# Preparing the first pair of chunks: norms from the token layout, 32x32 diagonal products of their own, beta applied after the inverse, and four banks for the second pair's gram products

## The chip, the cores and the metric

The kernel runs on one core of a Trainium2 chip. A core has a matrix engine (TensorE, PE in the profile), a vector engine (VectorE, DVE), a scalar engine (ScalarE, ACT), a general engine (GpSimd, POOL), and a fifth one that mostly issues transfers (SyncE, SP). Each runs its own list of instructions in order and waits on semaphores that the others raise. PE writes into eight PSUM banks of 128 x 512 floats; the other tiles lie in SBUF. The metric is the device time of one execution in microseconds (us), lower is better.

## The reference

Three stages: a delta-rule attention over 768 steps for 4 batches of 8 heads with head size 48, then two feed-forward stages over 3072 tokens.

```python
k_n = k / (np.linalg.norm(k, axis=-1, keepdims=True) + 1e-06)
for t in range(S):
    kt, vt, bt = (k_n[:, :, t], v[:, :, t], beta[:, :, t, None])
    y[:, :, t] = np.einsum('bhd,bhde->bhe', q[:, :, t], state)
    v_old = np.einsum('bhde,bhd->bhe', state, kt)
    state = state + bt[:, :, :, None] * np.einsum('bhd,bhe->bhde', kt, vt - v_old)
...
x = y.transpose(0, 2, 1, 3).reshape(B * S, H * D)
x = (x @ w_a) * (x @ w_b) @ w_out          # 384 -> 1536 -> 384
h = x @ w_in                               # 384 -> 2048
return (np.maximum(h, 0) + alpha * np.minimum(h, 0)) @ w_out2
```

## The kernel before

The sequence of 768 steps is cut into 12 chunks of T = 64 steps, handled in six pairs. Within a chunk the recurrence becomes a triangular system per head: the Gram products of the chunk's keys, scaled by beta, give a 64 x 64 matrix. The inverses of its 32 x 32 diagonal blocks are computed by VectorE alone, for all heads of both chunks at once: `IN` (a 32 x 32 block transpose `blk<-dgc`), 34 steps `ROW`, and `XT` (the transpose `xt<-inv`). After that the chain of small products `H2`, `H3`, `H4`, `HS`, `HY`, `H1` carries the state from chunk to chunk.

The rows of a pair's tokens for four batches form one tile of 512 tokens. The feed-forward stages of tile i run on PE as long three-part products (a high and a low half of each float), while the attention of pair i+1 is fitted in beside them. The first pair has no tile to lie beside: everything until the first unit `A` of tile 0 stands in front of it. This report is about that opening part.

One list, `seq`, holds the steps of the whole kernel in one order, and each engine walks through it and issues what is its own of every step. So the order of each engine's instructions is written by hand. The steps of the opening that the text speaks of:

- `LTK`, `LTQ` p b load keys and queries of pair p, batch b, with tokens on partitions and both heads of a pair side by side (`k_tok`, `q_tok`); `LK` loads keys in a second layout (`k_raw`), in which a chunk's tokens stand where the chain wants them. `WL` loads feed-forward weights.
- `SQ`, `KS`, `KN`, `KI` make the norms: square on ACT, sum on DVE, square root on ACT, and on DVE the reciprocal and its product with beta (`beta_all`).
- `BP`, `B` bring all beta values and alpha to partitions with 96 tiny products and one transpose on PE, and copy them out on ACT.
- `TRK`, `TRQ` transpose keys and queries of the first pair through the banks `att`, and ACT copies them to `kq0` and `kz0`. `TR` does the same for pair 1.
- `GK` c hf is the Gram product of the keys of chunk c, half hf of the heads; DVE multiplies it by beta into `gs`. `DG0` copies the 32 x 32 diagonal blocks out of `gs` to `dgc`, half on DVE, half on ACT. `GQ` is the product of keys and queries, `PT` its masking on DVE. `GG` c g makes both kinds for the chunks 2 and 3 of pair 1, in the two banks `att`; ACT copies them out.
- `VS` scales v by the norm on POOL. `GM` multiplies a `gs` by beta in place.
- `F` is a product of constants (`warm`), whose result nobody reads. It keeps PE busy.

PE and ACT work through `TR` and `GG` while DVE inverts; the chain's first product, `H2` of chunk 0, comes behind all of them in PE's list. A 32-bit product of the opening counts as two matmuls in the profile, a transpose and an `F` as one.

## Time and profile before

| | us |
|---|---|
| median of 3 runs | 1048.64 (1048.0 to 1048.91) |
| the profiled execution, its own time | 1048.36 |
| its span in the trace | 1046.6 |
| PE busy | 1020.3 (97% of the span) |
| DVE busy | 570.5 (55%) |
| ACT busy | 407.4 (39%) |
| first matmul of tile 0 | starts at 84.66 |

All times in the text are microseconds from the start of the span unless they are durations. An instruction's row gives its start, its time, its engine and line, what it writes and reads, how many instructions the row merges, and in brackets how long the engine sat idle before it and what ended that. PEclk is the granted share of the full clock of PE: 1.00 is 2.4 GHz and 0.50 is 1.2 GHz. After 84.66 PE is busy nearly without a break until the end.

### The profile page before, as it was taken

The page shows a single profiled execution, that of the slowest core. Times are in us where ns is not written, and L with a number is a line of the kernel's source. Part 1 is how long each engine was busy: PE and PEld are TensorE (multiplying, and loading weights), DVE is VectorE, ACT ScalarE, POOL GpSimd, SP SyncE. Part 2 cuts the span into 40 slices and gives each one's busy share as a digit, 9 for nine tenths or more (in the row PEclk, how much of TensorE's full clock was granted, in tenths as well). Part 3 has the DMA queues.
Part 4 walks back from the last instruction along what each step waited for, and adds up shares of the span by engine and source line. Part 5 has one row for each costly group of instructions (what it writes and reads, how often), then busy time and mean ns, then how long its engine had stood idle before and what let it go on. Part 6 is the DMA issues. An engine that isn't in the chain of part 4 may idle for free.

```text
span 1046.6 us, 24293 instructions
## 1 busy us (share of the span) xinstructions
PE 1020.3 (97%) x10240; PEld 853.1 (82%) x10240; DVE 570.5 (55%) x888; ACT 407.4 (39%) x774; POOL 113.5 (11%) x111
## 2 busy tenths in 40 slices
PE   6789999999999999999999999999999999999998
PEld 4557888898887888787889788889888888888898
DVE  5975876544687343496445477544368643322333
ACT  4425335564313344422434332435432334312433
POOL 4013663441000000000001000001000000000000
PEclk9899999999999999999999999999999999999999
DMA  9627998778875556696457596556556446766562
GB/s 159 127 64 224 305 325 265 240 247 277 223 228 168 164 166 218 182 251 185 147 159 233 157 249 208 154 167 205 173 177 194 144 150 185 224 194 195 182 191 81
DMA packets 191739, 203.82 MB, mean 195 GB/s; under 512 B 109392, under 2 KB 139168, under 8 KB 191632
## 3 DMA queue, kind: packets, MB, share of 16 engines
q1 hardware_dynamic: 188000, 200.73, 64.7%
q8 instruction: 82, 1.34, 0.6%
q0 software_dynamic: 576, 0.93, 0.5%
q10 hardware_dynamic: 3056, 0.61, 0.3%
q14 instruction: 25, 0.20, 0.1%
HBM read 166.04 MB, written 31.46 MB: 189 GB/s over the span
## 4 chain that ended last, share of the span: by engine, by line
PE 93%; ACT 3%; DVE 1%; issue 1%; DMA 1%; ACTq 0%; SPq 0%; DVEq 0%
PE bank L470 28%; PE bank L472 27%; PE bank L471 27%; PE bank L555 2%; PE bank L499 1%; PE bank L653 1%; PE bank L574 1%; PE bank L602 1%; PE bank L605 1%; PE bank L618 1%; PE bank L599 1%; ACT kz L770 1%; PE bank L647 1%; PE bank L650 1%; PE bank L563 1%
## 5 line engine op out<-in xcount | busy, mean ns | idle before, releaser
L877 ACT CAST g_hi<-g_sb 128x512 fp32r<-128x512 f32 x168 | 104.2, 620 | 249.2 <-DVE g_sb L1139 158.0
L470 PE MATMUL bank<-x_hi,w_two 128*128 128x512 f32 x432 | 171.2, 396 | 1.1 <-DVE x_lo L1128 1.1
L1144 DVE SCALAR_TENSOR_TENSOR g_sb<-f_sb,neg_alpha,e_sb 128x512 f32<-128x512 f32 x96 | 73.5, 766 | 177.7 <-ACT f_sb L874 177.0
L472 PE MATMUL bank<-x_hi,w_two 128*128 128x512 f32 x432 | 168.5, 390 | 0.0
L471 PE MATMUL bank<-x_lo,w_two 128*128 128x512 f32 x432 | 168.5, 390 | 0.0
L1150 DVE TENSOR_TENSOR g_lo<-g_sb,g_hi 128x512 fp32r<-128x512 f32 x168 | 121.0, 720 | 79.4 <-ACT g_hi L877 79.1
L472 PE MATMUL bank<-w_two,g_lo 128*128 128x384 f32 x384 | 129.2, 337 | 0.0
L470 PE MATMUL bank<-w_two,g_hi 128*128 128x384 f32 x384 | 129.1, 336 | 0.0
L471 PE MATMUL bank<-w_two,g_hi 128*128 128x384 f32 x384 | 128.8, 335 | 0.0
L1139 DVE TENSOR_TENSOR g_sb<-e_sb,bank 128x512 f32<-128x512 f32 x72 | 49.4, 686 | 140.8 <-PE bank L472 140.5
L470 PE MATMUL bank<-m_hi,w_two 128*128 128x512 f32 x288 | 118.1, 410 | 0.1
L471 PE MATMUL bank<-m_lo,w_two 128*128 128x512 f32 x288 | 113.6, 394 | 0.0
L472 PE MATMUL bank<-m_hi,w_two 128*128 128x512 f32 x288 | 113.2, 393 | 0.0
L873 ACT ACTIVATE e_sb<-bank 128x512 f32<-128x512 f32 x96 | 57.4, 598 | 132.5 <-PE bank L472 132.4
L866 ACT COPY e_sb<-bank 128x512 f32<-128x512 f32 x72 | 42.4, 588 | 149.0 <-PE bank L472 148.9
L470 PEld LDWEIGHTS bank<-x_hi,w_two 128*128 128x128 f32 x432 | 81.1, 188 | 19.1 <-issue 2.9
L472 PEld LDWEIGHTS bank<-x_hi,w_two 128*128 128x128 f32 x432 | 81.1, 188 | 17.2
L471 PEld LDWEIGHTS bank<-x_lo,w_two 128*128 128x128 f32 x432 | 81.2, 188 | 15.9
L1212 POOL TENSOR_TENSOR w_two<-w_ring,w_two 128x384 fp32r<-128x384 f32 x68 | 79.6, 1187 | 92.5 <-ACT w_two L853 92.4
L470 PE MATMUL bank<-g_hi,w_two 128*128 128x512 f32 x216 | 85.8, 397 | 0.3 <-DVE g_lo L1150 0.3
L471 PE MATMUL bank<-g_lo,w_two 128*128 128x512 f32 x216 | 84.3, 390 | 0.0
L472 PE MATMUL bank<-g_hi,w_two 128*128 128x512 f32 x216 | 84.2, 390 | 0.0
(143 smaller groups left out, 1536.5 us busy)
## 6 DMA issues: line engine op xcount, KB each, us to landing
w_two<-split_scratch SPq DMA_DIRECT2D x340, 384.0 KB, 3.5
split_scratch<-w_two SPq DMA_DIRECT2D x68, 384.0 KB, 4.3
w_ring<-in_moe_w_out_dram SPq DMA_DIRECT2D x28, 192.0 KB, 4.0
k_tok<-in_k_dram SPq DMA_DIRECT2D x24, 192.0 KB, 4.8
q_tok<-in_q_dram SPq DMA_DIRECT2D x24, 192.0 KB, 4.7
out_dram<-o_sb SPq DMA_DIRECT2D x24, 192.0 KB, 3.5
w_ring<-in_moe_w_in_dram SPq DMA_DIRECT2D x16, 192.0 KB, 3.9
x_raw<-y_sb SPq DMA_DIRECT2D x30, 96.0 KB, 2.4
```

Source lines behind the costliest of these rows:

```text
L470: pe.matmul(dst, lhs_hi, rhs_hi, start=start, stop=False)
L471: pe.matmul(dst, lhs_hi, rhs_lo, start=False, stop=False)
L472: return pe.matmul(dst, lhs_lo, rhs_hi, start=False, stop=stop)
L499: mm = pe.transpose(bk[:, j, i], src[:, 2 * g + j].rearrange("p h t -> p (h t)"), ident[:])
L555: mm = pe.matmul(bk[hf][tok(hf, h), 2 * T * j:2 * T * (j + 1)].rearrange("p (i t) -> p i t", t=T), kt(p, hf, w, e, rows), both, start=True ...
L866: act.copy(e_sb[:, f % 2], h_bank[0][:, :]).then_inc(e_ok, 1)
L873: act.activation(e_sb[:, f % 2], h_bank[f % 2][:, :], ACT.Relu).then_inc(e_ok, 1)
L877: act.copy(g_hi[:, j % GR], g_sb[:, j % GR]).then_inc(gh_ok, 1)
L1139: dve.tensor_tensor(g_sb[:, j % GR], e_sb[:, f % 2], h_bank[1][:, :], ALU.mult).then_inc(g_ok, 1)
L1144: dve.scalar_tensor_tensor(g_sb[:, j % GR], f_sb[:, f % 2], neg_alpha[:, f:f + 1], e_sb[:, f % 2], ALU.mult, ALU.add).then_inc(g_ok, 1)
L1150: dve.tensor_tensor(g_lo[:, s], g_sb[:, s], g_hi[:, s].bitcast(F32), ALU.subtract).then_inc(gl_ok, 1)
L1212: pool.tensor_tensor(w_lo[:, r], w_raw[:, r], w_hi[:, r].bitcast(F32), ALU.subtract).then_inc(lo_ok, 1)
```

## The change

- Norms of the first pair come from `k_tok`, by new steps `KS0` on DVE (square and sum, batch by batch as it lands), and `KP` on PE, which brings the sums to the chunk layout with 12 small products; `KN` takes the root from PSUM. `k_raw` of pair 0 is loaded later, behind the second pair's `LTQ`, and all of it by SP. The loads of `k_tok` and `q_tok` of pair 0 are shared by SP and ACT; POOL issues beta's.
- `GD` makes the 32 x 32 diagonal blocks by 128 products of their own (64 for each half), and `DG0` is now one DVE multiply by beta for each half, from PSUM to `dgc`. ACT copies the `GK` results to `gs` without beta, and `GM` 0 and 1 put beta in behind the inverse.
- `BP0` brings beta of the first two chunks only. The other 80 products of `BP`, alpha's transpose and the copies `B` move behind `GQ`.
- `GG` for chunk 3 uses two further banks (`spare`), and the six `F` between `GG` steps go. Sixteen `F` stand before `H2` of chunk 0, in four groups that wait for a step of the inverse each and for ACT's last copy from `spare`.
- `PT` of the first pair moves behind `H3` of chunk 0 and `H2` of chunk 1 in DVE's list, and `GM` 1 stands before DVE's part of `H1` of chunk 1.
- Two memsets of banks on DVE go, and one of `su` moves from DVE to POOL.

The diff, cut to its core:

```diff
+        spare, kn_bank, b0_bank = (bank[0], bank[2]), bank[3], bank[5]
...
-        seq = [("LK", 0, 0)] + [("LTK", 0, b) for b in range(B)] + [("LTQ", 0, b) for b in range(B)]
-        seq += [("BP",)] + [("F", 0)] * 8 + flat(norms(0)[:2]) + [("B",)] + flat(norms(0)[2:])
-        seq += [("TRK", 0)] + [("F", 0)] * 3 + [("TRK", 1)] + [("F", 0)] * 3 + [("GK", 0, 0), ("GK", 1, 0)]
-        seq += [("TRK", 2), ("TRK", 3)] + [("F", 0)] * 3 + [("DG0", 0), ("GK", 0, 1), ("GK", 1, 1), ("DG0", 1), ("IN", 0)]
+        seq = [("LTK", 0, b) for b in range(B)] + [("LTQ", 0, b) for b in range(B)]
+        seq += [("F", 3)] * 8 + [("KS0", 0), ("TRK", 0), ("F", 3), ("F", 3), ("KS0", 1), ("TRK", 1), ("BP0",), ("GD", 0)]
+        seq += [("KS0", 2), ("KS0", 3), ("TRK", 2), ("TRK", 3), ("KP",), ("KN", 0), ("GK", 0, 0), ("GD", 1), ("GK", 1, 0)]
+        seq += [("GK", 0, 1), ("GK", 1, 1), ("KI", 0), ("DG0", 0), ("DG0", 1), ("IN", 0)]
         seq += [("LTK", 1, b) for b in range(B)] + [("LTQ", 1, b) for b in range(B)]
-        seq += [("LK", 1, 0), ("LK", 1, 1)] + [("WL", n) for n in range(RG)] + [("VS", 0), ("VS", 1)]
-        seq += [("TRQ", b) for b in range(B)] + [("GQ", 0), ("GQ", 1), ("GC",)]
+        seq += [("LK", p, j) for p in range(2) for j in range(2)] + [("WL", n) for n in range(RG)] + [("VS", 0), ("VS", 1)]
+        seq += [("TRQ", b) for b in range(B)] + [("GQ", 0), ("GQ", 1), ("GC",), ("BP",), ("B",)]
         for g in TR_ORDER:
-            seq += [("TR", 1, g)] + [("F", 0)] * (2 * (g >= 4))
+            seq += [("TR", 1, g)] + [("F", 3)] * (2 * (g >= 4))
         for g in range(2):
             for c in (2, 3):
-                seq += [("GG", c, g)] + [("F", 0)] * (2 if (c, g) == (3, 1) else 6)
+                seq += [("GG", c, g)]
         seq += [("SQ", 2)]
         for n in range(1, ROWS + 1):
             seq += [("ROW", 0, n)]
-        seq += [("XT", 0)] + [("F", R16 + 14)] * 4 + [("F", ROWS)] * 8
-        seq += [("PT", 0, 0), ("PT", 0, 1)]
-        beside0 = {(0, "H2"): [("KS", 2), ("SQ", 3)], (0, "H4"): [("KS", 3), ("KN", 1)], (0, "HS"): [("KI", 1), ("LV", 2)],
-                   (0, "HY"): [("XL", 0, 0, T)], (1, "H1"): [("PT", 1, 0), ("PT", 1, 1), ("WS", 0)], (1, "H2"): [("WS", 1)],
-                   (1, "H3"): [("WS", 2)], (1, "H4"): [("GM", 2), ("GM", 3), ("WS", 3), ("WT", 0), ("WT", 1)]}
+        seq += [("XT", 0)] + [("F", 0, R16 + 8)] * 4 + [("F", 0, R16 + 12)] * 4 + [("F", 0, R16 + 14)] * 4 + [("F", 0, ROWS)] * 4
...
+        seq += [("GM", 0)]
+        beside0 = {(0, "H2"): [("KS", 2), ("SQ", 3)], (0, "H3"): [("PT", 0, 0), ("PT", 0, 1)], (0, "H4"): [("KS", 3), ("KN", 1)],
+                   (0, "HS"): [("KI", 1), ("LV", 2)], (0, "HY"): [("XL", 0, 0, T), ("GM", 1)], (1, "H1"): [("WS", 0)],
+                   (1, "H2"): [("PT", 1, 0), ("PT", 1, 1), ("WS", 1)], (1, "H3"): [("WS", 2)],
+                   (1, "H4"): [("GM", 2), ("GM", 3), ("WS", 3), ("WT", 0), ("WT", 1)]}
...
+                    if p == 0 and b % 2:
+                        continue
                     if p == 1:
                         sp.wait_ge(*is_full(b % 2, "TRK" if kind == "LTK" else "TRQ", b))
+                        if kind == "LTK":
+                            sp.wait_ge(ks0_ok, b + 1)
...
+                elif kind == "GD":
+                    hf = st[1]
+                    for b in range(2):
+                        pe.wait_ge(*is_free(b, "TRK", 2 * hf + b))
+                    for j in range(UH):
+                        for c in range(2):
+                            n = SB * (UH * c + j)
+                            for i in range(2):
+                                for h, rows in enumerate(LOW):
+                                    x = kt(0, hf, j, c, rows)[:, SB * i:SB * i + SB]
+                                    mm = pe.matmul(spare[hf][quad(2 * (h ^ hf) + i), n:n + SB], x, x, start=True, stop=True)
+                    mm.then_inc(gd_full, 1)
+                elif kind == "BP0":
+                    pe.wait_ge(beta_ld, 32)
+                    for c in range(2):
+                        mm = beta_quarters(b0_bank, c)
+                    mm.then_inc(b0_full, 1)
+                elif kind == "KP":
+                    pe.wait_ge(ks0_ok, B)
+                    for c in range(2):
+                        for h in range(2):
+                            pe.matmul(kn_bank[tok(0, h), c * U:c * U + UH], ident[:, c * T:c * T + T], ksum_tok[:, units(0), h],
+                                      start=True, stop=True)
+                            for i in range(2):
+                                mm = pe.matmul(kn_bank[quad(2 * (1 - h) + 1 - i), c * U + UH:c * U + U],
+                                               ident[:, c * T + SB * i:c * T + SB * i + SB], ksum_tok[:, units(1), h],
+                                               start=True, stop=True)
+                    mm.then_inc(kp_full, 1)
...
+                    if (c, hf) == (1, 0):
+                        pe.wait_ge(b0_ok, 1)
+                    elif (c, hf) == (1, 1):
+                        pe.wait_ge(kn_ok, 1)
...
+                    pe.wait_ge(dgv_ok, 2)
...
+                    if c == 3:
+                        if g:
+                            pe.wait_ge(sp_free, 2)
+                        bk, filled = spare, (sp_full, sp_full)
+                    else:
+                        bk, filled = in_banks(*st), full
...
-                    pe.wait_ge(vinit, 3)
                     if st[1]:
-                        pe.wait_ge(solve, st[1] + 1)
-                    pe.matmul(bank[0][:, :], warm[:, 0:P], warm[:], start=True, stop=True)
+                        pe.wait_ge(vinit, 2)
+                    else:
+                        pe.wait_ge(sp_free, 4)
+                        pe.wait_ge(solve, st[2] + 1)
+                    pe.matmul(bank[st[1]][:, :], warm[:, 0:P], warm[:], start=True, stop=True)
...
+                    if kind == "H3" and c < 2:
+                        pe.wait_ge(gm0_ok, c + 1)
...
-            for h in range(2):
-                act.dma_start(beta_rows[:, :, HALVES[h]], beta.rearrange("b (u two) (c t) -> two (b u) c t", two=2, t=T)[h]
-                              ).then_inc(beta_ld, 16)
-            load_k(act, 0, 1)
+            for kind in ("LTK", "LTQ"):
+                for b in range(1, B, 2):
+                    load_tok(act, kind, 0, b)
...
+                elif kind == "GK":
+                    _, c, hf = st
+                    act.wait_ge(gk_full, 2 * hf + c + 1)
+                    act.copy(gs(c)[:, units(hf), :].rearrange("p w t -> p (w t)"), g0_bank[2 * c + hf][:, :]).then_inc(gk_free, 1)
...
-                elif kind == "DG0":
-                    hf = st[1]
-                    act.wait_ge(gk_free, 2 * hf + 2)
-                    for i in range(2):
-                        for c in range(2):
-                            ins = act.copy(dgc[quad(i), c * U + UH * hf:c * U + UH * hf + UH, :],
-                                           gs(c)[quad(i), units(hf), SB * i:SB * i + SB])
-                    ins.then_inc(dg_ok, 1)
...
-            for x in y0_bank:
-                dve.memset(x[:, :], 0.0)
...
+                if kind == "KS0":
+                    b = st[1]
+                    dve.wait_ge(kt_ld[b], 16)
+                    x = k_tok[:, UQ * b:UQ * b + UQ, :, 0:D]
+                    dve.tensor_tensor(squares0(b), x, x, ALU.mult).then_inc(sq0_ok, 1)
+                    dve.wait_ge(sq0_ok, b + 1)
+                    dve.tensor_reduce(ksum_tok[:, UQ * b:UQ * b + UQ], squares0(b), AX.X, ALU.add).then_inc(ks0_ok, 1)
+                elif kind == "TRK" and st[1] == 3:
+                    dve.wait_ge(*is_full(1, *st))
+                    src = att[1][:, :].rearrange("p (w e t) -> p w e t", e=2, t=T)
+                    for i in range(2):
+                        ins = dve.tensor_copy(kz0[:, UQ:UH, :, 0, SB * i:SB * i + SB], src[:, :, :, SB * (1 - i):SB * (1 - i) + SB])
+                    ins.then_inc(free[1], 1)
...
+                    if c < 2:
+                        dve.wait_ge(gk_free, 4)
+                        dve.tensor_tensor(gs(c)[:], gs(c)[:], beta_all[:, c].unsqueeze(2).to_broadcast([P, U, T]), ALU.mult
+                                          ).then_inc(gm0_ok, 1)
+                        continue
...
-                elif kind == "GK":
-                    _, c, hf = st
-                    dve.wait_ge(gk_full, 2 * hf + c + 1)
+                elif kind == "DG0":
+                    hf = st[1]
+                    dve.wait_ge(gd_full, hf + 1)
                     dve.wait_ge(ki_ok, 3)
-                    dve.tensor_tensor(gs(c)[:, units(hf), :], g0_bank[2 * c + hf][:, :].rearrange("p (w t) -> p w t", t=T),
-                                      beta_all[:, c, units(hf)].unsqueeze(2).to_broadcast([P, UH, T]), ALU.mult
-                                      ).then_inc(gk_free, 1)
-                elif kind == "DG0":
-                    hf = st[1]
-                    dve.wait_ge(gk_free, 2 * hf + 2)
-                    for i in (2, 3):
-                        for c in range(2):
-                            ins = dve.tensor_copy(dgc[quad(i), c * U + UH * hf:c * U + UH * hf + UH, :],
-                                                  gs(c)[quad(i), units(hf), SB * (i - 2):SB * (i - 2) + SB])
-                    ins.then_inc(dgv_ok, 1)
+                    dve.tensor_tensor(dgc[:].rearrange("p (c u) t -> p c u t", c=2)[:, :, units(hf)],
+                                      spare[hf][:, :].rearrange("p (c u t) -> p c u t", c=2, t=SB),
+                                      beta_all[:, 0:2, units(hf)].unsqueeze(3).to_broadcast([P, 2, UH, SB]), ALU.mult
+                                      ).then_inc(dgv_ok, 1)
...
-            pool.dma_start(alpha_rows[:], alpha.rearrange("(f p) -> f p", p=P)).then_inc(al_ld, 16)
+            for h in range(2):
+                pool.dma_start(beta_rows[:, :, HALVES[h]], beta.rearrange("b (u two) (c t) -> two (b u) c t", two=2, t=T)[h]
...
-            pool.wait_ge(gk_full, 2)
+            pool.wait_ge(gq_full, 1)
```

The program's list of PE from its start up to the transposes of the queries, before (L538 and L541 are `BP`, L563 `F`, L508 `TRK` and `TRQ`, L516 `GK`):

```order
L538 MATMUL bank<-ident,y_sb 32x8 x96
L541 MATMUL bank<-ident,alpha_rows 128x16
L563 MATMUL bank<-warm 128x512 x8
L508 MATMUL bank<-ident,k_tok 128x128 x4
L563 MATMUL bank<-warm 128x512 x3
L508 MATMUL bank<-ident,k_tok 128x128 x4
L563 MATMUL bank<-warm 128x512 x3
L516 MATMUL bank<-kq 64x64 x32
L508 MATMUL bank<-ident,k_tok 128x128 x8
L563 MATMUL bank<-warm 128x512 x3
L516 MATMUL bank<-kz 64x64 x32
L508 MATMUL bank<-ident,q_tok 128x128 x16
```

The same stretch of PE's list in the changed program (L494 is `BP0`, L546 `GD`, L558 and L561 `KP`, L575 `GK`, L533 the transposes, L629 `F`):

```order
L533 MATMUL bank<-ident,k_tok 128x128 x4
L494 MATMUL bank<-ident,y_sb 32x8 x16
L546 MATMUL bank<-kq 32x32 x64
L533 MATMUL bank<-ident,k_tok 128x128 x8
L558 MATMUL bank<-ksum_tok,ident 64x8
L561 MATMUL bank<-ksum_tok,ident 32x8 x2
...
L575 MATMUL bank<-kq 64x64 x16
L546 MATMUL bank<-kz 32x32 x64
L575 MATMUL bank<-kq 64x64 x16
L575 MATMUL bank<-kz 64x64 x32
L533 MATMUL bank<-ident,q_tok 128x128 x16
```

The 96 products of `BP` have left the head of the list but for 16; `GD` and `KP` add 140 between the first transposes and the queries' ones.

DVE's list from the last transpose of the inverse on, before (L977 is `XT`, L1067 and L1073 `PT`, L1085 `H2`, L988 `KS`, L1099 `H3`, L1105 `H4`):

```order
L977 STREAM_TRANSPOSE xt<-inv 128x32x32
L1067 TENSOR_TENSOR pt_0<-bank,upper 128x512
L1073 TENSOR_TENSOR kz<-bank,upper 64x8x64 x2
L1085 COPY w_sb<-bank 128x384
L988 TENSOR_REDUCE ksum<-k_sq 128x16
L1099 TENSOR_TENSOR r_sb<-r_sb,bank 128x384 x2
L1105 TENSOR_TENSOR u_sb<-bank,beta_all 128x384
```

And in the changed program (L1049 is `XT`, L1099 `GM`, L1175 `H2`, L1073 `KS`, L1189 `H3`, L1157 and L1163 `PT`, L1195 `H4`):

```order
L1049 STREAM_TRANSPOSE xt<-inv 128x32x32
L1099 TENSOR_TENSOR gs_0<-gs_0,beta_all 128x1024
L1175 COPY w_sb<-bank 128x384
L1073 TENSOR_REDUCE ksum<-k_sq 128x16
L1189 TENSOR_TENSOR r_sb<-r_sb,bank 128x384 x2
L1157 TENSOR_TENSOR pt_0<-bank,upper 128x512
L1163 TENSOR_TENSOR kz<-bank,upper 64x8x64 x2
L1195 TENSOR_TENSOR u_sb<-bank,beta_all 128x384
```

`PT` has moved from before the chain into it, between `H3` and `H4`, and `GM` 0 stands where `PT` was.

PE's list behind `GQ` in the changed program (L494 and L598 are `BP`, L523 `TR`); before, the `TR` rows followed `GQ` directly:

```order
L588 MATMUL bank<-kz 64x64 x2
L494 MATMUL bank<-ident,y_sb 32x8 x80
L598 MATMUL bank<-ident,alpha_rows 128x16
L523 MATMUL bank<-ident,k_tok 128x2x64
L523 MATMUL bank<-ident,q_tok 128x2x64
```

The 80 products now stand between the last product of the first pair and everything that pair 1 needs.

## Rows read from the trace of the kernel before

**Rows 1.** The page: span, and the queue of instruction blocks (blocks, MB, share).
```profile
span 1046.6 us, 24293 instructions
...
q8 instruction: 82, 1.34, 0.6%
```

**Rows 2.** DVE in order of time: start, time, what, idle before and its releaser.
```profile
22.41 1.97 DVE L920 STREAM_TRANSPOSE blk<-dgc 128x1024 f32<-128x1024 f32 x1 [0.28 <-ACT dgc L791]
...
49.61 2.09 DVE L977 STREAM_TRANSPOSE xt<-inv 128x1024 f32<-128x1024 f32 x1
51.62 0.64 DVE L1067 TENSOR_TENSOR pt<-bank,upper 128x512 f32<-128x512 f32 x1
52.28 1.39 DVE L1073 TENSOR_TENSOR kz<-bank,upper 64x512 f32<-64x512 f32 x2
...
59.63 0.56 DVE L1105 TENSOR_TENSOR u_sb<-bank,beta_all 128x384 f32<-128x384 f32 x1 [1.22 <-PE bank L605]
...
71.10 1.02 DVE L1099 TENSOR_TENSOR r_sb<-r_sb,bank 128x384 f32<-128x384 f32 x2 [1.43 <-PE bank L602]
...
74.81 2.34 DVE L1013 TENSOR_TENSOR gs<-gs,beta_all 128x1024 f32<-128x1024 f32 x2
```

**Rows 3.** PE in order of time, the opening.
```profile
4.54 2.74 PE L538 MATMUL bank<-ident,y_sb 16*32 16x8 f32 x192 [4.54 <-DMA y_sb<-in_beta_dram]
...
7.43 3.59 PE L563 MATMUL bank<-warm 128*128 128x512 bf16 x8
...
14.06 2.15 PE L516 MATMUL bank<-kq 48*64 48x64 f32 x64
...
32.22 0.37 PE L528 MATMUL bank<-kz 48*64 48x64 f32 x2 [2.83 <-issue]
...
33.27 0.47 PE L499 MATMUL bank<-ident,k_tok 128*128 128x128 f32 x1
...
51.68 3.19 PE L563 MATMUL bank<-warm 128*128 128x512 bf16 x14
54.81 0.88 PE L599 MATMUL bank<-r_sb,xt 32*32 32x48 f32 x64
...
70.76 0.36 PE L602 MATMUL bank<-w_sb,gs 32*32 32x48 f32 x12 [0.15 <-issue]
...
76.16 0.26 PE L650 MATMUL bank<-pt,u_sb 64*48 64x64 f32 x2 [0.24 <-issue]
```

**Rows 4.** ACT in order of time.
```profile
9.29 0.84 ACT L742 ACTIVATE k_sq<-k_raw 128x768 f32<-128x768 f32 x1 [2.31 <-DMA k_raw<-in_k_dram]
...
23.74 2.37 ACT L784 COPY kz<-bank 64x512 f32<-64x512 f32 x4 [0.32 <-PE bank L508]
...
40.90 0.74 ACT L770 COPY kz<-bank 64x256 f32<-64x256 f32 x2
...
51.77 0.37 ACT L808 COPY gs<-bank 128x256 f32<-128x256 f32 x1 [1.27 <-PE bank L555]
...
52.71 0.75 ACT L813 COPY kz<-bank 64x256 f32<-64x256 f32 x2
```

**Rows 5.** Stretches: busy us (count) of PE, PEld, DVE, ACT, POOL; PEclk, DMA, GB/s.
```profile
0.00:29.40 29.40, 20.19 (x471) 15.30 (x471) 18.26 (x41) 11.95 (x25) 11.27 (x28) 0.93 1.12 159
...
0.00:70.70 70.70, 53.14 (x1216) 36.44 (x1217) 53.40 (x88) 31.09 (x73) 16.65 (x33) 0.93 0.69 115
0.00:76.15 76.15, 56.77 (x1342) 38.62 (x1343) 57.35 (x95) 31.09 (x73) 18.09 (x34) 0.93 0.67 118
```

**Rows 6.** DMA queues in 8.4:8.6, 16.4:16.6, 28.8:29, 59.8:60: blocks, MB, share.
```profile
q8 instruction: 1, 0.02, 44.3%
...
q8 instruction: 1, 0.02, 45.5%
...
q8 instruction: 1, 0.02, 53.3%
...
q8 instruction: 1, 0.02, 28.8%
```

120 lines of the change are left out of this document (77 added, 43 removed).

## The prediction

> **What bounds the kernel now.** I read the page first, then the engines' rows in order of time from 0 to 90, then the stretches, then the DMA queues. PE is busy without a break from 84.66 on, and the change leaves every instruction after that point as it is. So only the start of tile 0 can move, and the end moves with it, one to one. The opening ends in a chain of small products whose first, `H2` of chunk 0, starts at 54.81 [rows 3]. Everything between that and 84.66 hangs on it.
>
> Two strands meet at `H2`. The first is DVE: the inversion starts at 22.41 with the transpose to `blk` and ends with `xt` at 51.70, 29.3 us in which DVE waits for nobody [rows 2]. The second is PE and ACT in turn: `TR` from 33.27 [rows 3], ACT's last `TR` copy at 41.64, and four rounds of `GG`, of which ACT has the last copied out at 53.46 [rows 4]. PE then works off 14 `F` from 51.68 to 54.8 [rows 3]. `H2` starts as the last `F` ends, 3.1 us after `xt` is there. So the second strand is the later one: from the start of `TR` to `H2` it takes 54.81 - 33.27 = 21.5 us. The reader should also see the halt of 2.83 us at 32.22, within `GQ`, which the trace lays to "issue" [rows 3]: PE waited for no engine there, and it delays `TR` in full.
>
> **That halt is the key of this forecast.** Three PE rows of the opening have an idle time laid to "issue": 32.22, 70.76 and 76.16 [rows 3]. The matmuls recorded before them are 471, 1216 and 1342 [rows 5]. The distances are 745 and 126; 745 is 6 times 124. The page has 82 instruction blocks fetched [rows 1], and 10240 matmuls over 82 is 125. So PE's program comes in blocks of about 125 matmuls (each with its weight load), and the halts fall on the borders between blocks. Blocks are fetched by the same DMA engines as the data. Borders lie near matmul 98 (within `BP`, 4.54 + 98 x 2.74/192 = 5.9), 223 (14.3), 350 (19.9) and 471 (29.4). Block transfers start at about 8.5, 16.5, 28.9 [rows 6]: 2.5, 2.1 and 9.0 us behind the first three borders. The share of the stretch times 0.2 times 16 gives their lengths: 1.4, 1.5, 1.7. The halt ended at 32.22, 1.6 after the third transfer. This fits a fetch that is asked for at one border and needed at the next. From asking to having it took 2.5 + 1.4 + 1.6 = 5.5, then 5.2, then 12.3 us. Later, with the DMA engines nearly idle, the border at 58.7 has its transfer at 59.9, 0.9 long [rows 6]: 1.2 + 0.9 + 1.6 = 3.7 us. A block must therefore last 4 to 5 us, or PE stands still. The kernel before has one such halt, because its 193 matmuls of `BP` come first and `F` and waits stretch the rest.
>
> The Trainium skill ("Runtime: NRT & Kernel Launch", Instruction fetch mechanics) says blocks have 256 instructions, are fetched while the previous one runs, and that crossing a border is "mostly hidden"; it gives PE room for eight blocks. The block size agrees with this trace (125 matmuls and as many loads); the hiding does not, at 32.22, with its 2.83 us. By the skill's rule the halts would all be absent; the first rival below is that case.
>
> **The change part by part.** Start of the inversion. `F` runs from about 2.7 (the memsets of two banks, 1.0 us, are gone from DVE), 3.6 us for eight [rows 3]; the first transposes and two `F` end at 9.0. The keys have 192-byte pieces as before, where ACT had all of `k_raw` at 9.29 behind beta [rows 4]; now they are first in two queues, so about 5 to 8: no wait. `GD` 0 starts at 9.8. One `GK` pair of 64 matmuls takes 2.15 [rows 3]; `GD` has 128 matmuls, of a kind the trace does not show. `BP` gives 14.3 ns each, `H2` (32x32) 13.8, `GK` 34; `GD` uses four parts of the array at once like `H2`, so I take 14.3: 1.8 us for each half, 1.7 to 4.3 as bounds. Norms take DVE 4 x 1.1 us beside this and end at about 10. Without halts `GD` 1 ends at 15.9 and the inversion starts at 16.7, 5.7 us sooner than 22.41.
>
> With borders at the same spacing, they fall in the changed program at matmul 96 (the 46th of `GD` 0), 223 (13 matmuls into `GK`), 348 (the 106th of `GD` 1), 474 (the end of the second `TRQ`), 598 (near the end of `GQ`) and 724 (the 114th of the 160 of `BP`).
> - First border 9.8 + 46 x 0.0143 = 10.4. The DMA engines carry keys and queries as they did at 8.5. Block ready 5.5 later, 15.9, against 13.5 without a halt.
> - Second border 15.9; by then the loads have run dry (SP waits for `TRQ`), so 3.7: 19.6, against 18.1. `GD` 1 ends at 19.9 and the inversion starts at 21.0, `xt` is ready at 50.3.
> - From 19.6: rest of `GD` 1 0.3, three `GK` 3.2, `TRQ` with ACT's copies (two of 0.59, then 2.37 for four [rows 4]) to 27.7, `GQ` up to the 598th matmul 1.8: fifth border at 29.5. The one between, at 24.1, was asked for at 19.6 and costs nothing.
> - At 29.5 queries of pair 1, `k_raw` and v are in flight. Block ready 5.2 later (the second fetch of before; 3.7 to 12.3 as bounds): 34.7. Without a halt that border comes at 31.7. Then the rest of `BP`, alpha and ACT's `B`: 1.6.
> - `TR` starts at 36.3, against 33.27: +3.0 us. With no halts at all it would start at 28.6, since `BP` itself puts 2.4 us and `B` 0.5 in front of it.
>
> From `TR` to `H2`. Before 21.5. `TR` is ACT's time, 8.3 from 33.27 to 41.64. `GG` before took 11.8, from 41.64 to 53.46; with four banks ACT's copies follow each other, 1.70 each (51.77 to 53.46 [rows 4]), 4 x 1.70 + 1.1 for the first product + 0.1 of gaps = 8.0. The sixteen `F` wait for the last of them (`sp_free` 4): 16 x 3.13/14 = 3.6 us, all behind it, since three of their four steps of the inverse are past. Sum 8.3 + 8.0 + 3.6 = 19.9, so -1.6 us. `H2` is then at 56.2, behind `xt` (50.3) and `GM` 0, which is hidden.
>
> From `H2` to tile 0. `PT` stands between `H3` and `H4` on DVE: it frees at 58.4 (59.63 less the idle 1.22), plus 2.03 for `PT` [rows 2] is 60.5, against 59.63: +0.85. In chunk 1 `GM` 1 (2.34 / 2 = 1.17) and `PT` stand in front of `r_sb`; `PT` has left the place before `w_sb`, and the step at 71.10 comes at 71.7: +0.6. Together +1.45; bounds 0 (if the loads before tile 0 cover it) and 3.2 (2.03 + 1.17, all in series).
>
> Sum: +3.0 - 1.6 + 1.45 = +2.85 us. The profiled execution took 1048.36, of which the span is 1046.6, so 1051.2; it lay 0.3 under the median of the runs, so I say 1051.4.
>
> **Rivals.**
> - A: no halts. For: between 40 and 84 the halts are 0.24 at most [rows 3]. Against: 32.22. `TR` at 28.6 is -4.7, with -1.6 and +1.45 makes -4.85: 1043.8. (This is the case of the rule quoted from the Trainium skill.) If `GD` and the small products run still quicker, 1042.5.
> - B: short halts, 3.7 us for every block. Second border 14.1, third 17.8, `GQ`'s 27.6, `BP` continues at 31.3, `TR` at 32.9: -0.4 - 1.6 + 1.45 = -0.5: 1048.1. No measurable change.
> - C, slower: my forecast. It decides from the point where the three exposed fetches sum to over 12 us (`TR` later than 33.4); here 5.5 + 3.7 + 5.2 = 14.4.
> - D: a fetch behind `GQ` like the third of before, 12.3 us, with PE at half clock in `TR` after the halt: `TR` at 43.4, +10: 1058.
> - E: `k_raw` of pair 1 lands late, 24 loads being issued by SP alone after `LTQ`. I expect them by 48 and ACT's square after 52; it costs nothing unless PE runs without halts, then up to 1 us.
>
> **How the numbers follow.** 0.43 for C with 1049.8 to 1055, 0.03 for D, 0.22 for B (within 0.2%, 2.1 us, which is about what a measurement of this kernel can tell from no change) and 0.32 for A with what lies between it and B. C's own range is 1049.5 to 1055.5. For all, the range is 1043.4 to 1055.3: A's end leaves out about a tenth, D and the far end of C another. Faster 0.32, same 0.22, slower 0.46. The likeliest single case is C, 1051.4.
>
> **What would show it.** In the changed profile: idle times laid to "issue" of 1 to 3 us in `GK` (L575) after 13 matmuls and late in the second `GD` (L546), and one of 3 us or more within the 160 matmuls of L494; the inversion's transpose at 21 (not 16.7); `TR` at 36; ACT's `GG` copies back to back; sixteen `F` in one piece of 3.6 us before `H2`. I am wrong if the halts are missing or under 1 us in sum, if `TR` starts before 31, or if `F` is spread over the inverse's steps, which would say that the second strand was ahead of DVE.

## The result, and the profile after

| | before | after |
|---|---|---|
| median of the runs made together | 1048.32 (4 runs, 1046.83 to 1048.91) | 1061.03 (4 runs, 1060.78 to 1061.81) |
| ratio, 95% interval | | 1.0125 (1.0107 to 1.0142) |
| span of the profiled execution | 1046.6 | 1059.0 |
| first matmul of tile 0 | 84.66 | 97.41 |

The change makes the kernel slower by 1.25%. The forecast was 1051.4, with 1043.4 to 1055.3 as range: the sign came out, and halts for instruction blocks are there as forecast, but the size did not come out, and the result lies outside the range. From tile 0 to the end both need the same time (961.9 and 961.6), so the whole loss is in the opening. Split at the points that the prediction uses:

| us | before | after | difference | forecast |
|---|---|---|---|---|
| start of `TR` | 33.27 | 41.00 | +7.7 | +3.0 |
| from there to the first `GG` | 8.5 | 9.1 | +0.6 | 0 |
| from there to ACT's last `GG` copy | 11.7 | 7.6 | -4.1 | -3.8 |
| from there to `H2` of chunk 0 | 1.4 | 5.8 | +4.4 | +2.2 |
| from there to tile 0 | 29.85 | 33.99 | +4.1 | +1.45 |
| sum | 84.66 | 97.41 | +12.75 | +2.85 |

PE of the changed kernel in order of time (the columns are those of [rows 3], which these rows answer):

```profile
12.86 0.50 PE L575 MATMUL bank<-kq 48*64 48x64 f32 x9
16.66 1.54 PE L575 MATMUL bank<-kq 48*64 48x64 f32 x23 [3.30 <-issue]
18.14 1.64 PE L546 MATMUL bank<-kz 48*32 48x32 f32 x105
20.22 0.54 PE L546 MATMUL bank<-kz 48*32 48x32 f32 x23 [0.44 <-issue]
...
22.41 2.83 PE L575 MATMUL bank<-kz 48*64 48x64 f32 x58
...
29.98 0.27 PE L588 MATMUL bank<-kq 48*64 48x64 f32 x2 [2.27 <-ACT kz L864]
...
34.48 0.37 PE L588 MATMUL bank<-kq 48*64 48x64 f32 x2 [2.14 <-issue]
...
35.12 1.68 PE L494 MATMUL bank<-ident,y_sb 16*32 16x8 f32 x112
39.40 0.83 PE L494 MATMUL bank<-ident,y_sb 16*32 16x8 f32 x48 [2.61 <-issue]
...
41.00 0.45 PE L523 MATMUL bank<-ident,k_tok 128*128 128x128 f32 x1 [0.56 <-ACT neg_alpha L815]
...
57.72 5.77 PE L629 MATMUL bank<-warm 128*128 128x512 bf16 x16 [1.74 <-ACT kz L888]
63.42 0.88 PE L667 MATMUL bank<-r_sb,xt 32*32 32x48 f32 x64
...
72.34 1.95 PE L723 MATMUL bank<-kz,su 128*48 128x64 f32 x32
...
84.01 0.88 PE L673 MATMUL bank<-r_sb,xt 32*32 32x48 f32 x64 [2.59 <-DVE r_sb L1189]
```

The reader sees four halts laid to "issue" in place of the one of before: 3.30 behind the ninth of the first `GK`, 0.44 behind the 105th of the second `GD`, 2.14 in `GQ`, 2.61 behind the 112th of the late `BP`. Together 8.5 us. Three stand where the block borders were forecast (13th, 106th, 114th matmul). The sixteen `F` take 5.77 us, not 3.6.

The granted clock in four stretches (PE, PEld, DVE, ACT, POOL busy with counts; PEclk; DMA share; GB/s), against which before has 1.00 until 22 and from 38 on:

```profile
14.00:18.00 4.00, 1.34 (x23) 1.33 (x22) 0.96 (x3) 0.00 (x0) 0.00 (x0) 0.54 0.86 124
18.00:22.00 4.00, 3.56 (x154) 3.25 (x155) 1.08 (x2) 0.58 (x1) 0.00 (x0) 0.50 0.02 4
...
38.00:42.00 4.00, 2.04 (x54) 1.94 (x55) 3.79 (x7) 0.38 (x2) 1.12 (x2) 0.50 0.85 161
...
58.00:62.00 4.00, 4.00 (x11) 1.36 (x10) 0.00 (x0) 0.41 (x1) 0.00 (x0) 0.50 0.04 9
```

DVE, answering [rows 2]. The inversion starts at 21.61, and its second half of diagonals had waited 5.71 us for PE:

```profile
20.82 0.69 DVE L1147 TENSOR_TENSOR dgc<-bank,beta_all 128x512 f32<-128x512 f32 x1 [5.71 <-PE bank L546]
21.61 1.95 DVE L992 STREAM_TRANSPOSE blk<-dgc 128x1024 f32<-128x1024 f32 x1
...
48.88 2.11 DVE L1049 STREAM_TRANSPOSE xt<-inv 128x1024 f32<-128x1024 f32 x1
...
79.55 0.68 DVE L1157 TENSOR_TENSOR pt<-bank,upper 128x512 f32<-128x512 f32 x1
80.26 2.67 DVE L1163 TENSOR_TENSOR kz<-kz,upper 64x512 f32<-64x512 f32 x2
82.86 1.00 DVE L1189 TENSOR_TENSOR r_sb<-r_sb,bank 128x384 f32<-128x384 f32 x2
```

ACT's copies of `GG` ([rows 4]) now follow one another, and the last ends at 57.66:

```profile
51.20 0.37 ACT L883 COPY gs<-bank 128x256 f32<-128x256 f32 x1 [1.27 <-PE bank L618]
...
56.92 0.74 ACT L888 COPY kz<-bank 64x256 f32<-64x256 f32 x2
```

### The profile page after: what moved, and what is told of

The parts are those of the page before. It is cut to its first block, busy times and chain, and to the rows that moved or that the text cites. A ratio compares the mean times of both kernels' runs of the same rounds, so it can differ in the third digit from the quotient of the medians.

```text
span 1059.0 us, 24861 instructions
## 1 busy us (share of the span) xinstructions
PE 1025.0 (97%) x10497; PEld 859.2 (81%) x10497; DVE 572.9 (54%) x885; ACT 404.4 (38%) x768; POOL 117.8 (11%) x114
## 4 chain that ended last, share of the span: by engine, by line
PE 93%; ACT 2%; issue 2%; DVE 1%; DMA 1%; SPq 0%; POOL 0%; DVEq 0%; ACTq 0%; POOLq 0%
PE bank L486 28%; PE bank L488 26%; PE bank L487 26%; PE bank L618 2%; PE bank L523 1%; PE bank L723 1%; PE bank L640 1%; PE bank L667 1%; PE bank L688 1%; PE bank L673 1%; PE bank L670 1%; PE bank L629 1%; ACT kz L850 1%; PE bank L717 1%; DMA y_sb<-in_beta_dram 1%
```

## The experiments

Every time of a milestone below is from the profiled execution of its kernel. The kernel before was run beside each set: medians of 1048.52, 1047.01, 1047.72 and 1047.57 us. Its 13 runs beside the first set lie between 1046.06 and 1051.61, so a difference of 1 or 2 us between kernels that ran once says little by itself; there the milestones within the trace carry the argument.

**Do halts move with the number of products?** Three kernels add work to the kernel before. In two of them the added product is one of `BP`'s kind, in the third an `F`, and nobody reads what they write. All diffs below are cut to the lines of `seq` and the few others that matter.

b_shift, 32 tiny products in front (64 recorded matmuls, half a block):

```diff
-        seq += [("BP",)] + [("F", 0)] * 8 + flat(norms(0)[:2]) + [("B",)] + flat(norms(0)[2:])
+        seq += [("SM", 4), ("BP",)] + [("F", 0)] * 6 + flat(norms(0)[:2]) + [("B",)] + flat(norms(0)[2:])
```

> The kernel before with 32 more tiny products (64 matmuls) in front of BP and two F fewer; 62 matmuls are added ahead of everything. Theory 1 (a block of about 125 matmuls is asked for at one border and needed at the next): the halt within GQ moves from the 101st recorded matmul of GQ to about the 40th, and the two small halts of H3 and HY in chunk 1 move about 62 matmuls earlier too. Theory 2 (the halts belong to a place or a time, such as the loads of v or a bank in use): the halt stays at the same product of GQ or at the same time, 29.4. The time changes by less than 2 us either way.

Measured 1053.33 (one run), tile 0 at 89.74. The halt in `GQ` is gone, and a new one stands in `BP`, behind its 158th matmul, which is the 222nd of the program, where the second border lies:

```profile
5.46 2.32 PE L538 MATMUL bank<-ident,y_sb 16*32 16x8 f32 x158
11.14 0.65 PE L538 MATMUL bank<-ident,y_sb 16*32 16x8 f32 x34 [3.35 <-issue]
```

The little halts of [rows 3] moved too, about 60 matmuls to the front. So a halt belongs to a place in the instruction stream. Whether there is one, and how long, depends on how soon PE gets there: here 222 tiny matmuls are over within 3.2 us, and before the same border was passed at 14.3 without a halt. Two things were not as the first theory had them: no halt stands at the 40th matmul of `GQ`, and the time grew by some 5 us (tile 0 by 5.1) and not by under 2.

b_small80, 80 tiny products between `GQ` and `TR`, where the change puts the late `BP`:

```diff
-        seq += [("TRQ", b) for b in range(B)] + [("GQ", 0), ("GQ", 1), ("GC",)]
+        seq += [("TRQ", b) for b in range(B)] + [("GQ", 0), ("GQ", 1), ("GC",), ("SM", 10)]
```

> The kernel before with 80 tiny products (160 matmuls, the same kind as BP) between GQ and TR, where the changed kernel has BP. Their own time is 2.3 us. Theory 1: they use up more than a block within 2.3 us, so a further halt of 2 to 5 us appears inside them at about the 97th matmul; TR starts 4.5 to 7 us later than 33.3. Theory 2 (only the time in PE's list counts): TR starts 2.3 us later and no halt appears.

b_long6, six `F` in the same place:

```diff
+        seq += [("TRQ", b) for b in range(B)] + [("GQ", 0), ("GQ", 1), ("GC",)] + [("F", 0)] * 6
```

> The kernel before with six F in the same place as the 80 tiny products of the other run: 6 matmuls instead of 160, at 0.22 to 0.43 us each 1.3 to 2.6 us of PE time. Theory 1: no new halt, TR starts 1.3 to 2.6 us later. Theory 2 expects the same here as for the 80 products, some 2.3 us.

b_small80 took 1052.37, with tile 0 at 88.67. It has the halt in `GQ` and a further one within the added products:

```profile
32.07 0.37 PE L528 MATMUL bank<-kz 48*64 48x64 f32 x2 [2.28 <-issue]
...
35.90 1.02 PE L549 MATMUL bank<-ident,y_sb 16*32 16x8 f32 x60 [1.22 <-issue]
```

`TR` starts at 36.85, 3.6 later than before. The further halt stands where it was expected, but with 1.22 it is shorter than the 2 to 5 us expected, and so is the delay of `TR` (4.5 to 7). b_long6 took 1047.56, with tile 0 at 84.00 and `TR` at 32.84. Its trace has no halt in `GQ` at all, although this lies in front of the edit. That was not expected. The position of the instructions is the same, so the halt of 2.83 us on which the prediction was built comes and goes between executions. The six `F` were not free: from the start of `GQ` to `TR` b_long6 took 6.2 us, and b_f2 (below), which has no halt there either and no added `F`, 3.6. They cost 2.5 us at half clock, about what the missing halt gave back, and brought no further halt.

**Which strand sets `H2` in the kernel before?** b_f2 has 2 `F` instead of 14 in front of it:

```diff
-        seq += [("XT", 0)] + [("F", R16 + 14)] * 4 + [("F", ROWS)] * 8
+        seq += [("XT", 0)] + [("F", ROWS)] * 0
```

> The kernel before with 2 instead of 14 F ahead of H2 of chunk 0 (3.13 us of PE). xt is ready at 51.7 and PE is done with GG at 51.8, ACT at 53.5. H2 needs both banks free and so starts at about 53.5 instead of 54.8. Theory: 1.3 us faster (0.1%), unless PE falls to half clock in the chain, which would cost some 1 to 3 us.

Ratio 0.9993 (0.9982 to 1.0004), no measurable change where 1.3 us were expected. Its profiled execution again has no halt in `GQ`, and `H2` waits for the inversion:

```profile
52.80 0.88 PE L599 MATMUL bank<-r_sb,xt 32*32 32x48 f32 x64 [2.65 <-DVE xt L977]
```

The two strands of before end within 1 to 3 us of each other, and without the halt DVE is the later one. The prediction called PE and ACT the later strand: true for the execution it had, not for all. `H2` starts 2.0 us sooner than before, tile 0 only 0.6 (84.09): without the `F` the granted clock is 0.54 from 54 to 58 and 0.61 from 58 to 62, where before has 1.00.

b_gg4 takes one part of the change alone to the kernel before, the four banks for `GG`, with 2 `F` in front of `H2`:

```diff
-                seq += [("GG", c, g)] + [("F", 0)] * (2 if (c, g) == (3, 1) else 6)
+                seq += [("GG", c, g)]
...
+                    if c == 3:
+                        if g:
+                            pe.wait_ge(sp_free, 2)
+                        bk, filled = spare, (sp_full, sp_full)
+                    else:
+                        bk, filled = in_banks(*st), full
```

> The kernel before with one part of the change alone: four banks for the Gram products of pair 1, without the F between them, and 2 F instead of 14 in front of H2. From the start of GG to ACT's last copy 7.7 us instead of 11.8. As the inversion ends at 51.7 to 52.7 whatever PE does, and the kernel with 2 F alone already waited for it, the theory (both strands end together in the kernel before) expects no measurable change: 1046 to 1048, ratio 0.998 to 1.001, H2 waiting 3 us or more for DVE. Rival (the second strand alone sets H2, the inversion has slack): H2 4 us sooner, 1043 to 1044.

Median 1046.40 (11 runs), ratio 0.9988 (0.9979 to 0.9997). `GG` takes 8.2 us until the last copy at 48.88, `xt` is ready at 51.53 and `H2` starts at 51.64. The theory held: the part that works as forecast is worth a tenth of a per cent, since DVE is next. It is the fastest kernel of the study by its median, with a gain hardly larger than what can be told.

**The halts of the changed kernel, one by one.** a_k1late holds pair 1's keys back until the Gram products are done (`gk_full` 4):

```diff
                         if kind == "LTK":
                             sp.wait_ge(ks0_ok, b + 1)
+                            sp.wait_ge(gk_full, 4)
```

> The changed kernel with the keys of pair 1 loaded only after all four GK are done, so that no data load runs while PE asks for the blocks of GK and GD. Theory 1 with the DMA engines' load as the cause of the long fetch: the first fetch (asked for at about 9.6, ready at 16.7, 7.0 us) gets shorter by 1 to 3 us, since only the queries of pair 0 are still coming, the halt before GK's 14th matmul falls from 3.3 to 0.5 to 2 us, and the inversion starts at 18.5 to 20.5 instead of 21.6. Later fetches get longer, as the loads are moved there. Rival (a fetch takes 5 to 7 us whatever the loads do): the halt stays at 3 us.

1059.11 (one run). The first halt shrank from 3.30 to 1.57, as its block's transfer starts at 12.0 and not at 13.5, and the inversion starts at 19.81 and not at 21.61. The other halts are longer than in the changed kernel:

```profile
14.87 0.91 PE L576 MATMUL bank<-kq 48*64 48x64 f32 x23 [1.57 <-issue]
18.42 0.55 PE L547 MATMUL bank<-kz 48*32 48x32 f32 x23 [1.22 <-issue]
...
33.22 0.37 PE L589 MATMUL bank<-kq 48*64 48x64 f32 x2 [2.68 <-issue]
...
39.24 0.82 PE L495 MATMUL bank<-ident,y_sb 16*32 16x8 f32 x48 [3.71 <-issue]
```

Their sum is 9.2, against 8.5. How much of this is the edit? Five more kernels of this study have the same instructions up to `GQ` as the changed kernel, and the first three halts vary among these six without any cause in the program: 2.2 to 3.3, 0.4 to 1.4 and 1.3 to 2.7 us. The late `BP`'s halt is 1.8 to 3.2 in the four that have it at the same place. So 1.57 lies below its spread and 3.71 above, while 1.22 and 2.68 lie within. That data transfers in flight lengthen a fetch is suggested by the first halt, in one execution; that the harm was moved to the later ones is not shown. `TR` starts at 40.84, so the 1.9 us less in the time are not from there: the sixteen `F` ran at full clock (58.19 to 61.74, 3.6 us).

a_gkdiag takes the diagonal products out again. The blocks are copied from `gs` as in the kernel before and multiplied by beta in `dgc`:

```diff
-        seq += [("F", 3)] * 8 + [("KS0", 0), ("TRK", 0), ("F", 3), ("F", 3), ("KS0", 1), ("TRK", 1), ("BP0",), ("GD", 0)]
-        seq += [("KS0", 2), ("KS0", 3), ("TRK", 2), ("TRK", 3), ("KP",), ("KN", 0), ("GK", 0, 0), ("GD", 1), ("GK", 1, 0)]
-        seq += [("GK", 0, 1), ("GK", 1, 1), ("KI", 0), ("DG0", 0), ("DG0", 1), ("IN", 0)]
+        seq += [("F", 3)] * 8 + [("KS0", 0), ("TRK", 0), ("F", 3), ("F", 3), ("KS0", 1), ("TRK", 1), ("BP0",), ("GK", 0, 0)]
+        seq += [("KS0", 2), ("KS0", 3), ("TRK", 2), ("TRK", 3), ("GK", 1, 0), ("DC", 0), ("KP",), ("KN", 0)]
+        seq += [("GK", 0, 1), ("KI", 0), ("GK", 1, 1), ("DC", 1), ("DG0", 0), ("DG0", 1), ("IN", 0)]
```

> The changed kernel without the 128 products of the diagonal blocks (256 recorded matmuls, two instruction blocks): the diagonals are copied out of the Gram matrices of the pair, half on ACT and half on DVE, as the kernel before did, and multiplied by beta in place on DVE. All else as in the changed kernel, 16 F too. Theory (PE halts because small products use up an instruction block sooner than the next is fetched): border 2 now falls into the transposes of the queries, no longer in front of the Gram products that the inversion waits for, so the inversion starts at 17 to 19 instead of 21.6; TR starts at 32 to 35 instead of 41.0, H2 of chunk 0 at 52 to 56 instead of 63.4, and the time is 1049 to 1054 instead of 1061. Rival (the halts are a matter of the transfers in flight, and not of the number of products in front): halts at the same times, 16.7 and 34.5, TR at 39 or later, and the extra copies on ACT and DVE bring the start of the inversion to 22 or later: 1060 or more.

1052.95 (one run), 8.1 under the changed kernel. DVE and PE:

```profile
17.87 1.29 DVE L1151 TENSOR_TENSOR dgc<-dgc,beta_all 128x512 f32<-128x512 f32 x2
19.27 1.95 DVE L987 STREAM_TRANSPOSE blk<-dgc 128x1024 f32<-128x1024 f32 x1
```

```profile
26.40 0.37 PE L575 MATMUL bank<-kq 48*64 48x64 f32 x2 [1.31 <-issue]
...
31.33 0.82 PE L494 MATMUL bank<-ident,y_sb 16*32 16x8 f32 x47 [2.58 <-issue]
...
32.92 0.45 PE L523 MATMUL bank<-ident,k_tok 128*128 128x128 f32 x1 [0.56 <-ACT neg_alpha L802]
...
55.41 0.88 PE L654 MATMUL bank<-r_sb,xt 32*32 32x48 f32 x64
```

Both halts in front of the inversion are gone, it starts 2.3 us sooner in spite of the copies, and `TR` and `H2` start 8.1 and 8.0 us sooner. The 128 products, 3.5 us of PE by their rows (1.29 at 9.11, 1.64, 0.54), cost 8: the remaining 4.6 is what the halts fell by, from 8.5 in sum to 3.9.

**The late `BP`.** a_bplate puts it behind the last `GG`, a_f4 leaves it, and both have 4 `F` instead of 16 before `H2`:

```diff
-        seq += [("TRQ", b) for b in range(B)] + [("GQ", 0), ("GQ", 1), ("GC",), ("BP",), ("B",)]
+        seq += [("TRQ", b) for b in range(B)] + [("GQ", 0), ("GQ", 1), ("GC",)]
...
-        seq += [("SQ", 2)]
+        seq += [("BP",), ("B",), ("SQ", 2)]
...
+        seq += [("XT", 0)] + [("F", 0, ROWS)] * 4
```

> The changed kernel with BP and B moved from behind GQ to behind the last GG, and 4 instead of 16 F ahead of H2. Theory 1: TR starts without BP's 2.4 us, its halt of 2.6 and the wait for B (0.8), so at about 35.2 instead of 41.0; the halt in GQ stays. H2 starts at about 54 instead of 63.4 (5.8 from there, 3.5 from the F, less the clock). About 9 us faster than the changed kernel: 1052. Rival (BP's place is no matter, something else holds TR): TR stays near 41.

> The changed kernel with 4 instead of 16 F ahead of H2. They took 5.8 us at half clock, all of it exposed. Theory: 12 x 0.43 at first and 0.22 later gives 4 us less before H2; PE then runs the chain's first products at half clock, which gives 1 to 2 us back. H2 at about 59.4 instead of 63.4, the whole 2 to 4 us faster than the changed kernel. Rival: F keeps the clock that the chain needs, and the chain loses as much as the F cost; no gain.

a_f4: 1057.90 (one run); `H2` at 59.87, the four `F` 1.04 us. a_bplate: median 1057.08 (4 runs), ratio to before 1.0095 (1.0077 to 1.0112). `TR` starts at 34.61 and `GG` at 43.24, 6.4 and 6.8 us sooner than in the changed kernel, but the halt went along, and half clock with it:

```profile
48.79 0.73 PE L494 MATMUL bank<-ident,y_sb 16*32 16x8 f32 x63
53.04 1.50 PE L494 MATMUL bank<-ident,y_sb 16*32 16x8 f32 x97 [3.52 <-issue]
54.68 1.89 PE L629 MATMUL bank<-warm 128*128 128x512 bf16 x4
```

`H2` at 56.50. The move had been expected to bring 5 us more than it did. Against a_f4, which differs by the move alone, `H2` comes 3.4 us sooner, tile 0 only 1.7 (92.93 and 94.59) and the time 0.8: from `H2` to tile 0 it takes 36.4 and not 34.7, with PE at half clock at its start.

a_bpmix spreads these products over the first five `TR`, into a bank of their own (`BPM` n makes two chunks' worth; 4 `F`):

```diff
-            seq += [("TR", 1, g)] + [("F", 3)] * (2 * (g >= 4))
+            seq += [("TR", 1, g), ("BPM", TR_ORDER.index(g))] + [("F", 3)] * (2 * (g >= 4))
...
+                elif kind == "BPM":
+                    n = st[1]
+                    if n < 5:
+                        beta_quarters(spare[0], 2 + 2 * n)
+                        beta_quarters(spare[0], 3 + 2 * n)
```

> The changed kernel with 4 F instead of 16 in front of H2 of chunk 0, and with the 80 late products of beta taken apart: 16 of them after each of the first five TR, written to a bank of their own, so that they lie beside ACT's copies of TR. Theory of the blocks: the halt that fell into these products (2.6 to 3.7 us in the runs so far) falls between the TR, where PE has slack (ACT needs 8.5 us for TR, PE about 4 at full clock); TR starts at 34.5 to 35.5, GG at 43.5 to 45.5, H2 at 53 to 54.5: 1051 to 1053. Against the same with all of these products behind GG (1057.1, H2 at 56.5), that is 4 us sooner. Rival (the halt is as long in wall time wherever it stands, and TR alone cannot hide it because its own copies on ACT wait for PE): GG at 47 or later and 1056 or more.

1058.85 (one run), `GG` at 49.49: the theory fell here and the rival's number came out, for neither's reason. No halt in `TR` is over 0.33. But PE runs at half clock from 34 to 46, and ACT waits for it:

```profile
34.00:38.00 4.00, 3.40 (x64) 2.59 (x67) 3.86 (x5) 1.66 (x4) 4.00 (x7) 0.50 0.92 184
38.00:42.00 4.00, 3.67 (x85) 2.82 (x88) 3.76 (x8) 1.64 (x5) 0.70 (x2) 0.50 0.85 157
42.00:46.00 4.00, 4.00 (x76) 3.15 (x72) 3.90 (x4) 1.64 (x5) 0.00 (x0) 0.50 0.51 91
```

ACT is busy 1.64 of each 4 us, where it was the bound before. In the changed kernel the clock is back at 1.00 within 4 us from the start of `TR`; in the other executions with the same `TR` (a_ptback, a_pt1, a_k1late, a_f4) it takes 3.4 to 6.2, here about 12.

**From `H2` to tile 0.** a_ptback puts `PT` of both chunks and both `GM` in front of the chain (and takes them out of their places in it, lines not shown):

```diff
-        seq += [("GM", 0)]
+        seq += [("PT", 0, 0), ("PT", 0, 1), ("PT", 1, 0), ("PT", 1, 1), ("GM", 0), ("GM", 1)]
```

> The changed kernel with PT and both GM in front of the chain on DVE, as PT stood before. DVE has 11 us idle there. From H2 to the copy of y (88.86 less 63.42 = 25.4 us) it should take 22.9 as before: PT and GM 1 no longer stand in the chain, PE idles less and keeps its clock. 2.6 us faster than the changed kernel. Rival: the 2.6 us come from something else (POOL and DVE at the same port, the clock after the F), then most of it stays.

1060.32 (one run). `H2` at 63.38, as in the changed kernel; tile 0 at 95.19, 31.8 behind it and not 34.0. So 2.2 us of the 4.1 are `PT` and `GM` on DVE. Only 0.7 us show in the time, because early matmuls of tile 0, from the third on, ran at half clock, 1.8 us in all (0.63 a matmul and not 0.39).

a_pt1 puts `PT` of chunk 1 alone back to where it stood:

```diff
-                   (0, "HS"): [("KI", 1), ("LV", 2)], (0, "HY"): [("XL", 0, 0, T), ("GM", 1)], (1, "H1"): [("WS", 0)],
-                   (1, "H2"): [("PT", 1, 0), ("PT", 1, 1), ("WS", 1)], (1, "H3"): [("WS", 2)],
+                   (0, "HS"): [("KI", 1), ("LV", 2)], (0, "HY"): [("XL", 0, 0, T), ("GM", 1)], (1, "H1"): [("PT", 1, 0), ("PT", 1, 1), ("WS", 0)],
+                   (1, "H2"): [("WS", 1)], (1, "H3"): [("WS", 2)],
```

> The changed kernel with one move undone: PT of chunk 1 stands again in front of w_sb of chunk 1 on DVE, beside PE's H2. 16 F, halts and all else as in the changed kernel. If PT between w_sb and r_sb is what PE waits 2.6 us for in front of H4 of chunk 1, that wait shrinks to 0.4 to 0.6 and tile 0 starts 2 us sooner: from H2 to tile 0 31.5 to 32.3 instead of 34.0, time 1058.5 to 1059.5. Rival (DVE's list is full anyway, the wait only moves in front of H3): 34 us, 1061.

Median 1059.72 (4 runs), ratio 1.0111 (1.0097 to 1.0124); tile 0 at 97.34, 34.2 behind `H2`. The wait of 2.59 is 0.40 as expected, yet in the trace nothing is gained:

```profile
77.36 0.88 PE L667 MATMUL bank<-r_sb,xt 32*32 32x48 f32 x64 [1.55 <-DVE r_sb L1171]
...
81.12 0.53 PE L670 MATMUL bank<-w_sb,gs 32*32 32x48 f32 x28 [0.66 <-issue]
82.80 0.88 PE L673 MATMUL bank<-r_sb,xt 32*32 32x48 f32 x64 [0.40 <-DVE r_sb L1189]
...
86.78 0.27 PE L720 MATMUL bank<-pt,u_sb 64*48 64x64 f32 x4 [0.65 <-issue]
```

A microsecond of it moved in front of `H2` of chunk 1, and halts of 0.66 and 0.65 stand where the changed kernel has none. When PE's products in the chain come sooner, the blocks are late again: a_ptback has 0.94, 0.38 and 0.30 there. The trace is that of the slowest of the four runs (1060.84; two took 1058.79 and 1058.93). The median lies between the two expectations, and the interval overlaps that of the changed kernel (1.0107 to 1.0142), so whether the move is worth its 1 us or nothing is not decided.

**All together.** a_best has a_gkdiag, a_bpmix and a_ptback in one, with 4 `F`; a_best2 has a_gkdiag, a_bplate and a_pt1, with 4 `F`. Their diffs are those above.

> The changed kernel with four edits together: no products of their own for the diagonal blocks, 4 F instead of 16, the late products of beta spread between TR, and PT of both chunks and both GM in front of the chain on DVE. By the theory of the blocks: inversion starts at 17 to 19 and its result is there at 46.5 to 48.5; TR starts at 27 to 29, ACT has the last GG copied at 44 to 47; H2 at 47 to 49, waiting for DVE; tile 0 starts 30 to 31.5 later, at 77 to 80: 1039 to 1043, ratio to the kernel before 0.992 to 0.996. By the rival (the number of small products does not matter): inversion from 21.5 on, H2 at 51.5 or later, 1045 or more.

> The changed kernel without the products of their own for the diagonal blocks, with the 80 late products of beta and alpha behind the last GG, with 4 F instead of 16 in front of H2, and with PT of chunk 1 in front of w_sb (its place in the kernel before) instead of behind H2. Theory (small products use up instruction blocks, PT in the chain costs about 2 us, F and half clock the rest): inversion starts at 19 and xt is ready at 48.4; TR at 27, ACT has the last GG copied by 43.5; the late products have a halt of 2 to 4 us that lies under the inversion; H2 at 48.5 to 50, tile 0 at 31 to 32 us behind it: 80 to 82, time 1042 to 1045, ratio 0.994 to 0.998. Rival (the way from H2 to tile 0 is longer for another reason, PE's clock or the loads of x_raw, and PT has little to do with it): 34 us behind H2, 1046 to 1048.

a_best: ratio 1.0026 (1.0016 to 1.0037), median 1050.34 (8 runs; a ninth took 2545.72 and is left out), where 0.992 to 0.996 was expected. The inversion ends at 48.3 as expected, and `H2` starts at 49.51, half a microsecond behind the expected 47 to 49, at half clock. But `PT` and `GM` stand in front of the copy of its result on DVE:

```profile
49.51 1.50 PE L656 MATMUL bank<-r_sb,xt 32*32 32x48 f32 x64
...
55.16 1.50 PE L659 MATMUL bank<-w_sb,gs 32*32 32x48 f32 x64 [3.33 <-DVE w_sb L1181]
```

It was an oversight in the expectation: where the inversion is the later strand, nothing covers work that is put behind it. Tile 0 at 85.58, 36 behind `H2`.

a_best2: median 1048.11 (11 runs), ratio 0.9998 (0.9989 to 1.0008), where 0.994 to 0.998 was expected. `H2` at 48.39, 6.4 us sooner than before; tile 0 at 83.70, 35.3 behind it. Expected were 31 to 32. So the diagonal products, the place of the late `BP` and the `F` account for the loss up to `H2`, and more; the way from there stays long. By its rows, `H2` at half clock takes 1.50 and not 0.88, the chain's copies wait for `GM` 0, `PT` of chunk 0 is in the chain, halts are 0.47 and 0.68, and the clock falls within the first microseconds of tile 0:

```profile
82.00:86.00 4.00, 2.30 (x8) 1.92 (x9) 1.90 (x3) 1.66 (x3) 0.00 (x0) 0.88 0.62 161
86.00:90.00 4.00, 4.00 (x14) 3.13 (x13) 0.24 (x1) 2.13 (x4) 1.00 (x1) 0.69 0.41 147
```

## Why the prediction was wrong in size

**What held.** Blocks of 256 instructions (128 recorded matmuls, each with its weight load, lie between the first two halts and between the last two); halts at three of the places named; `GG` with four banks (7.6, forecast 8.0); the start of the inversion (21.61, forecast 21.0, though partly by luck: the first half of `GD` took 10.1 ns a matmul and not 14.3, so that its border was passed at 9.5 and not at 10.4, and the first fetch took 7.2 us and not 5.5); all `F` in one piece behind ACT's last copy; 3.6 us from asking for a block to having it while data transfers rest (16.66 to 20.22, forecast 3.7), and 4.9 behind `GQ` (34.48 to 39.40, forecast 5.2). Rivals A and B, with no or short halts, are out.

**First step that failed: the fifth border.** The prediction had PE at the border in `GQ` at 29.5 without a halt; it was passed at 34.48. The difference of 5.0 comes in three parts. The block in front was ready at 20.22 and not at 19.6. `GK` ran at half clock (the 58 matmuls at 22.41 took 2.83, before a pair of 64 took 2.15 [rows 3]), so that `GQ` began at 29.98 and not at 27.7, and `GQ` itself fell to half clock at 31.3: together some 2.2. The halt of 2.14 is the rest. The block of `GQ` had been priced as free, since it was asked for early; its transfer began at 31.6, though PE had been at the border before it by about 26.0: 8.5 us from asking to having. This step fails in the same way in all seven kernels that share these instructions, with 8.4 to 9.0 us. In the kernel before and its variants the third border shows a delay as long in three executions and none to speak of in two, so that one execution could not tell whether the 12.3 us that the prediction found there are the rule or the exception:

| kernel | third block's transfer starts | halt in `GQ` |
|---|---|---|
| before | 29.0 | 2.83 |
| b_small80 | 29.1 | 2.28 |
| b_gg4 | 27.7 | 1.73 |
| b_f2 | 21.8 | none |
| b_long6 | 20.7 | none |

PE passed the border before it at 19.6 to 20.8 in all five. Why a transfer starts at once in one execution and 8 to 9 us late in another is open. Data transfers in flight alone do not decide it: from 20 to 28 the DMA share is 1.2 to 1.4 in all five.

**Second: sixteen `F` at full clock.** They were priced by [rows 3], 3.13 for 14. The clock had fallen at 55.2, within the last `GG`, whose `F` the change takes away; PE then idled 1.74, the clock was at 0.5 until 62, and they took 5.77. It is not so in every execution: in a_ptback and a_pt1 the sixteen took 5.4 and 5.3, but in a_k1late 3.6. a_f4 shows what they cost: 3.1 us in the time for twelve `F` (one run).

**Third: from `H2` to tile 0, 1.45 against 4.1.** `PT` and `GM` in the chain are 2.2 (a_ptback), of which a part only shows because POOL's subtraction lies beside `PT` of chunk 1 (`kz` 2.67 and not 1.39, with POOL's `w_two` at 79.98 for 3.81). `HY` of chunk 0 at half clock is 0.85 (1.95 at 72.34; 1.10 at full clock). The rest, some 1.5, lies between the copy of `y_sb` of chunk 1 and tile 0: 8.4 us, before 6.9. The last `x_raw` that POOL issues and the last of SP landed 4.3 and 4.2 us behind their issue, before 2.7 each. The changed loads of the opening are not the reason: b_small80, which has those of before, shows 3.9 for both. What goes with it is again an instruction block. In the changed kernel one is transferred from 93.0 to 94.0, between the issue of the last `x_raw` (91.7) and tile 0, and the same holds for b_small80 and all nine variants of the changed kernel. SP's last `x_raw` takes 3.9 to 4.5 in all of these whose trace has its landing. In before, b_f2, b_gg4, b_long6 and b_shift no block falls there, and it takes 1.9 to 2.8. No run moves that block alone, so this cause is argued and not shown. (The three overlap in part: 4.6 in sum, 4.1 measured.)

**What was not weighed at all** is that a halt costs more than its own length. Behind the halt of 3.30 the clock is at 0.50 (18 to 22), and behind those in `GQ` and `BP` again (34 to 42; in `GQ` it had fallen at 31.3 already, behind a wait of 2.27 for ACT); at half clock what had slack beside ACT has none, as a_bpmix shows.

The Trainium skill ("Runtime: NRT & Kernel Launch", Instruction fetch mechanics) gives PE room for eight blocks. The traces do not agree: in b_shift PE stands still from 7.8 to 11.1 at the second border, 222 matmuls into the program, and the transfer that ends this starts only at 8.2. Its block size agrees with the halts (128 matmuls and as many weight loads between them).

## What to carry to other kernels

Count the instructions of small products, not their microseconds: a block of 256 is over in 1.8 us when its products are tiny, and the next one took 3.6 to 12.3 us to come, so a few dozen products that look free can cost more than the copies they replace. Before work is moved out of one wait, look at which strand is next, and by how much, in more than one execution. A measured duration holds only at the clock at which it was measured: behind a halt of some microseconds, price what follows at half clock too.

## What the runs showed of the hardware that was not expected

- At the same border the block's transfer started 0.5 to 1.1 us behind PE's passing it in two kernels and 8 to 9 us in three (table above).
- With small products between the transposes PE stayed at half clock for 12 us from 34 on, busy 3.4 to 4.0 of every 4 us (a_bpmix); with transposes and `F` alone 1.00 was back 3.4 to 6.2 us from the start of `TR`.
- An idle time of 2.2 to 2.7 us in front of tile 0 went with half clock in its first microseconds in a_ptback, a_best and a_best2, 1.5 to 2.0 us lost, and not in five other kernels with 2.2 to 2.8, the changed one among them.
- Two DVE instructions on 64 partitions took 2.67 and not 1.39 while POOL subtracted beside them, in the changed kernel and five of its variants (a_bpmix 2.64); in a_pt1, where they end before POOL starts, they took 1.39.
